# Queries with keys and state sums in all four corners of TensorE, and three of the steps around them in other slots

## The reference

```
for t in range(S):
    kt, vt, bt = (k_n[:, :, t], v[:, :, t], beta[:, :, t, None])
    y[:, :, t] = np.einsum('bhd,bhde->bhe', q[:, :, t], state)
    v_old = np.einsum('bhde,bhd->bhe', state, kt)
    state = state + bt[:, :, :, None] * np.einsum('bhd,bhe->bhde', kt, vt - v_old)
...
h = x @ w_in
g = np.maximum(0.01 * h, h)
x = (g @ w_out)
...
e_idx = np.argmax(logits, axis=1)
out[mask] = gate_w[mask, None] * (np.maximum(x[mask] @ w1[e], 0.0) @ w2[e])
```

## Time and profile before

| | |
|---|---|
| median of three runs | 981.32 us |
| the three runs | 974.87, 981.32, 982.77 us |
| profiled execution | 978.93 us |
| its span, first to last instruction | 977.2 us |
| mean granted clock of PE | 0.957 |
| PE busy | 870.9 us |
| DVE busy | 553.5 us |
| ACT busy | 350.6 us |
| DMA, mean | 80 GB/s |

### The profile page before, as it was taken

The page is one execution under the profiler, slowest core; times in us unless marked ns, Lnnn a source line. Parts: engine busy times, 40 slices in busy tenths (PEclk is TensorE's granted clock), DMA queues, the critical chain, the costliest instruction groups (busy, mean ns, idle before and its releaser), DMA issues.

```text
span 977.2 us, 26906 instructions
## 1 busy us (share of the span) xinstructions
PE 870.9 (89%) x10528; PEld 766.0 (78%) x10529; DVE 553.5 (57%) x1578; ACT 350.6 (36%) x609; POOL 87.6 (9%) x100
## 2 busy tenths in 40 slices
PE   3775889989999998999989999999969999999962
PEld 3664678878888887888878888888759898889862
DVE  4974994588638862798359842344642333333350
ACT  3364335542545253444444342323411212121230
POOL 1000000000020002000100001010121212121210
PEclk9965899999999999999999999999999999999996
DMA  9904272345143533344153313255051111111122
GB/s 127 337 4 75 62 150 68 68 107 101 34 92 74 104 62 52 99 86 81 41 102 84 74 28 84 58 94 175 32 171 33 48 32 48 32 48 32 40 74 73
DMA packets 148308, 77.92 MB, mean 80 GB/s; under 512 B 112496, under 2 KB 144240, under 8 KB 147824
## 3 DMA queue, kind: packets, MB, share of 16 engines
q1 hardware_dynamic: 143264, 66.59, 30.4%
q0 software_dynamic: 4096, 9.48, 3.2%
q10 hardware_dynamic: 848, 0.39, 0.2%
HBM read 59.30 MB, written 13.21 MB: 74 GB/s over the span
## 4 chain that ended last, share of the span: by engine, by line
PE 67%; DVE 15%; ACT 7%; DMA 4%; issue 3%; SPq 1%; ACTq 1%; DVEq 0%; POOL 0%; POOLq 0%
PE bank L518 17%; PE bank L503 14%; PE bank L605 11%; PE bank L580 10%; DVE inv_t L1299 2%; DVE inv_tmp L1293 2%; PE bank L590 2%; PE bank L381 2%; PE bank L410 2%; ACT diag L987 2%; DVE g_raw L1368 1%; PE bank L484 1%; DVE tr L1305 1%; PE bank L471 1%; DVE inv_a L1255 1%
## 5 line engine op out<-in xcount | busy, mean ns | idle before, releaser
L518 PE MATMUL bank<-wo_hi,g_hi 128*128 128x392 f32 x384 | 139.1, 362 | 7.3 <-DVE g_lo L1373 4.0
L518 PE MATMUL bank<-wo_hi,g_lo 128*128 128x392 f32 x384 | 132.2, 344 | 0.0
L518 PE MATMUL bank<-wo_lo,g_hi 128*128 128x392 f32 x384 | 132.1, 344 | 0.0
L1368 DVE SCALAR_TENSOR_TENSOR g_raw<-g_raw 128x512 f32<-128x512 f32 x96 | 66.3, 691 | 105.0 <-ACT g_raw L1043 105.0
L503 PE MATMUL bank<-x_hi,wi_hi 128*128 128x512 f32 x288 | 118.3, 411 | 6.2 <-ACT g_raw L1043 3.4
L1043 ACT ACTIVATE g_raw<-bank 128x512 f32<-128x512 f32 x96 | 57.3, 597 | 170.5 <-PE bank L503 170.1
L503 PE MATMUL bank<-x_hi,wi_lo 128*128 128x512 f32 x288 | 114.0, 396 | 0.0
L503 PE MATMUL bank<-x_lo,wi_hi 128*128 128x512 f32 x288 | 113.9, 395 | 0.0
L1050 ACT ACTIVATE g_hi<-g_raw 128x512 fp32r<-128x512 f32 x96 | 60.7, 632 | 116.9 <-DVE g_raw L1368 116.9
L1373 DVE TENSOR_TENSOR g_lo<-g_raw,g_hi 128x512 fp32r<-128x512 f32 x96 | 66.3, 691 | 41.9 <-ACT g_hi L1050 41.7
L518 PEld LDWEIGHTS bank<-wo_hi,g_hi 128*128 128x128 f32 x384 | 72.7, 189 | 13.8 <-issue 6.0
(11 more groups left out here) (215 smaller groups left out, 1493.3 us busy)
## 6 DMA issues: line engine op xcount, KB each, us to landing
wo_lo<-wo_lo_d SPq DMA_DIRECT2D x80, 196.0 KB, 2.4
w_raw<-in_moe_w SPq DMA_DIRECT2D x6, 1536.0 KB, 8.4
x_rows<-stage SPq DMA_DIRECT2D x6, 770.0 KB, 6.2
kq_in_rows<-in_k SPq DMA_DIRECT2D x6, 768.0 KB, 7.0
k_raw<-in_k SPq DMA_DIRECT2D x24, 192.0 KB, 4.0
vals<-in_v SPq DMA_DIRECT2D x48, 96.0 KB, 2.9
kq_in_rows<-in_q SPq DMA_DIRECT2D x6, 768.0 KB, 8.8
x_raw<-y_t SPq DMA_DIRECT2D x33, 96.0 KB, 2.4
```

What stands on the lines that cost most here:

```text
L518: mm = pe.matmul(acc[i][:, 0:DX], g[f % 2][:, P * i:P * i + P], w, start=(f == 0 and k == 0), stop=(f == FT - 1 and k == 2))
L1368: dve.scalar_tensor_tensor(out=g_raw[f % 2][:], in0=g_raw[f % 2][:], scalar=0.01, in1=g_raw[f % 2][:], op0=ALU.mult, op1=ALU.max).then_inc ...
```

## The change

- `gram_q(t, c)` does the 16 pairs of a chunk in one go, into two banks, in four corners; it stands in slot 15 (chunk 0) and at the head of slot 0, ahead of `up(n, 1)` (chunk 1), instead of slots 15, 0, 1 and 2.
- `state_sum(t, c)` does its 16 pairs in one go, in four corners; that of chunk 1 stands ahead of `down` in slot 12, where there was one half ahead of it and one behind.
- Odd pairs' results now lie in the other half of the partitions. So for odd pairs `mask_q` and `add_s` take two DVE instructions of 64 partitions each, which read one half of the bank and write the other half of the tile.
- `add_s` of chunk 1 stands ahead of `norm` on DVE, `mask_q` of chunk 1 in slot 0.
- The queries' third and fourth transposes stand behind `down` in slot 13 instead of in slot 14, and their copies behind the first two on ACT.

```diff
--- before.py
+++ after.py
@@ -400,16 +400,17 @@
                                       beta_rows[:, c, :, :].rearrange("p a b -> p (a b)"), ident[:PAIRS, :PAIRS])
                 mm.then_inc(s.beta_tp, 1)
 
-            def gram_q(t, m):
-                for i in range(2):
-                    pe.wait_ge(*is_drained(("QT", t, m % 2 * 2 + i)))
-                b, done = fill(("QK", t, m))
+            def gram_q(t, c):
+                for m in range(4):
+                    pe.wait_ge(*is_drained(("QT", t, m)))
+                to = [fill(("QK", t, c, odd)) for odd in range(2)]
                 for j in range(8):
-                    pair = m % 2 * 8 + j
-                    for hh in range(2):
-                        mm = pe.matmul(b[half_p(hh), CH * j:CH * j + CH], k_t[head_p(hh), pair, chunk(m // 2)],
-                                       q_t[head_p(hh), pair, chunk(m // 2)], start=True, stop=True)
-                mm.then_inc(done, 1)
+                    for odd in range(2):
+                        for hh in range(2):
+                            mm = pe.matmul(to[odd][0][half_p(hh ^ odd), CH * j:CH * j + CH], k_t[head_p(hh), 2 * j + odd, chunk(c)],
+                                           q_t[head_p(hh), 2 * j + odd, chunk(c)], start=True, stop=True)
+                        if j == 7:
+                            mm.then_inc(to[odd][1], 1)
 
             def merge_x(t, m):
                 pe.wait_ge(s.tr_ready, t + 1)
@@ -459,22 +460,24 @@
                         if j == 7:
                             mm.then_inc(to[odd][1], 1)
 
-            def state_sum(t, c, m):
-                if c == 0 and m == 0:
+            def state_sum(t, c):
+                if c == 0:
                     pe.wait_ge(s.k_in, 64 * t + 64)
                 for odd in range(2):
                     pe.wait_ge(*is_drained(("U", t, c, odd)))
-                b, done = fill(("S", t, c, m))
+                to = [fill(("S", t, c, odd)) for odd in range(2)]
                 for j in range(8):
-                    g = 16 * c + 8 * m + j
-                    for hh in range(2):
-                        mm = pe.matmul(b[head_p(hh), HD * j:HD * j + HD], k_raw[half_p(hh), g, :], u_sb[half_p(hh), g, :],
-                                       start=True, stop=True)
-                mm.then_inc(done, 1)
+                    for odd in range(2):
+                        g = PAIRS * c + 2 * j + odd
+                        for hh in range(2):
+                            mm = pe.matmul(to[odd][0][head_p(hh ^ odd), HD * j:HD * j + HD], k_raw[half_p(hh), g, :], u_sb[half_p(hh), g, :],
+                                           start=True, stop=True)
+                        if j == 7:
+                            mm.then_inc(to[odd][1], 1)
 
             def outputs(t, c):
                 for m in range(2):
-                    pe.wait_ge(*is_drained(("QK", t, 2 * c + m)))
+                    pe.wait_ge(*is_drained(("QK", t, c, m)))
                     pe.wait_ge(*is_drained(("U", t, c, m)))
                 to = [fill(("Y", t, c, odd)) for odd in range(2)]
                 for j in range(8):
@@ -614,14 +617,14 @@
 
             def slot(n, f):
                 cur, nxt, ff = is_set(n + 1), is_set(n + 2), n >= 0
+                if cur and f == 0:
+                    gram_q(n + 1, 1)
                 if ff and f < FT - 1:
                     up(n, f + 1)
                 if n == -1 and f == 13:
                     pe.wait_ge(s.beta_cp, 1)
                     up(0, 0)
                 if cur:
-                    if f < 3:
-                        gram_q(n + 1, f + 1)
                     if f == 5:
                         merge_x(n + 1, 0)
                         merge_x(n + 1, 1)
@@ -641,16 +644,13 @@
                     if f == 11 and n >= 0:
                         outputs(n + 1, 1)
                     if f == 12:
-                        state_sum(n + 1, 1, 0)
+                        state_sum(n + 1, 1)
                 if n >= 1 and f == (3 if n == TT - 1 else 8):
                     ranks(n - 1)
                 if nxt:
                     if f == 13:
                         queries_t(n + 2, 0)
                         queries_t(n + 2, 1)
-                    if f == 14:
-                        queries_t(n + 2, 2)
-                        queries_t(n + 2, 3)
                     if f == 15:
                         gram_q(n + 2, 0)
                 if n == -1 and f == 4:
@@ -668,10 +668,7 @@
                     if f == 5 and n >= 0:
                         old_values(n + 1, 0)
                     if f == 7:
-                        state_sum(n + 1, 0, 0)
-                        state_sum(n + 1, 0, 1)
-                    if f == 12:
-                        state_sum(n + 1, 1, 1)
+                        state_sum(n + 1, 0)
                 if nxt:
                     if f == 8:
                         keys_t(n + 2, 0)
@@ -685,6 +682,9 @@
                         gram_k(n + 2, 0)
                     if f == 11:
                         gram_k(n + 2, 1)
+                    if f == 13:
+                        queries_t(n + 2, 2)
+                        queries_t(n + 2, 3)
 
             pe.wait_ge(s.ident_rdy, 1)
             pe.wait_ge(s.pads_zero, 1)
@@ -1305,10 +1304,16 @@
                 dve.transpose(tr[:].rearrange("p g c -> p c g"), inv_t[:].rearrange("p i c -> p c i")).then_inc(s.tr_ready, 1)
                 dve.transpose(diag[:].rearrange("p g i -> p i g"), inv_t[:]).then_inc(s.tt_ready, 1)
 
-            def mask_q(t, m):
-                dve.wait_ge(*is_filled(("QK", t, m)))
-                dve.tensor_tensor(qk_t[:, eight(m), :], by_8(att_bank(("QK", t, m))[:]),
-                                  mask[:].unsqueeze(1).broadcast_to([P, 8, CH]), ALU.mult).then_inc(drain(("QK", t, m)), 1)
+
+            def halves(odd):
+                return [(half_p(hh), half_p(1 - hh)) for hh in range(2)] if odd else [(slice(0, P), slice(0, P))]
+
+            def mask_q(t, c, odd):
+                dve.wait_ge(*is_filled(("QK", t, c, odd)))
+                for to, at in halves(odd):
+                    mm = dve.tensor_tensor(qk_t[to, every_other(c, odd), :], by_8(att_bank(("QK", t, c, odd))[at, :]),
+                                           mask[at, :].unsqueeze(1).broadcast_to([to.stop - to.start, 8, CH]), ALU.mult)
+                mm.then_inc(drain(("QK", t, c, odd)), 1)
 
             def scale_v(t):
                 dve.wait_ge(s.v_in, 128 * t + 128)
@@ -1333,10 +1338,12 @@
                 x = vals[:, every_other(c, odd), :]
                 dve.tensor_tensor(x, x, by_48(att_bank(("W", t, c, odd))), ALU.subtract).then_inc(drain(("W", t, c, odd)), 1)
 
-            def add_s(t, c, m):
-                dve.wait_ge(*is_filled(("S", t, c, m)))
-                old, new = (state[i][:, eight(m), :].rearrange("p a b -> p (a b)") for i in (c, 1 - c))
-                dve.tensor_tensor(new, old, att_bank(("S", t, c, m))[:, 0:8 * HD], ALU.add).then_inc(drain(("S", t, c, m)), 1)
+            def add_s(t, c, odd):
+                dve.wait_ge(*is_filled(("S", t, c, odd)))
+                old, new = state[c], state[1 - c]
+                for to, at in halves(odd):
+                    mm = dve.tensor_tensor(new[to, odd::2, :], old[to, odd::2, :], by_48(att_bank(("S", t, c, odd))[at, :]), ALU.add)
+                mm.then_inc(drain(("S", t, c, odd)), 1)
 
             def split_wi(p):
                 dve.wait_ge(s.wih, p + 1)
@@ -1547,14 +1554,16 @@
                 for i in inv[:len(inv) // 2]:
                     inverse(inv_set, i)
                 if cur:
-                    if f < 3:
-                        mask_q(n + 1, f + 1)
+                    if f == 0:
+                        mask_q(n + 1, 1, 0)
+                        mask_q(n + 1, 1, 1)
                     if f == 5:
                         copy_x(n + 1, 0)
                     if f == 8:
                         sub_w(n + 1, 1, 0)
                 if nxt and f == 15:
-                    mask_q(n + 2, 0)
+                    mask_q(n + 2, 0, 0)
+                    mask_q(n + 2, 0, 1)
                 if ff and f < FT - 1:
                     rest_g(n, f + 1)
                 if 0 <= n < TT - 1 and f == 14:
@@ -1571,6 +1580,9 @@
                         add_s(n + 1, 0, 1)
                     if f == 8:
                         sub_w(n + 1, 1, 1)
+                if cur and f == 12:
+                    add_s(n + 1, 1, 0)
+                    add_s(n + 1, 1, 1)
                 if nxt:
                     if f == 10:
                         copy_gram(n + 2, 0, 1)
@@ -1580,9 +1592,6 @@
                         if n == -1:
                             split_x(0)
                         norm(n + 2)
-                if cur and f == 12:
-                    add_s(n + 1, 1, 0)
-                    add_s(n + 1, 1, 1)
                 for i in inv[len(inv) // 2:]:
                     inverse(inv_set, i)
                 if cur and f == 4:
```

## The result

| | before | after |
|---|---|---|
| median | 981.32 us | 985.82 us |
| lowest to highest of 15 runs | 973.99 to 985.42 | 980.79 to 992.01 |
| ratio, with its 95% interval | | 1.0066 [1.0037, 1.0095] |
| span of the profiled execution | 977.2 us | 979.1 us |
| mean granted clock of PE | 0.957 | 0.940 |

The kernel is 0.7% slower, some 6.5 us by the ratio. The two profiled executions differ by 1.9 us of span alone, but the expert layer, which the change doesn't touch, took 282.1 us in the one after and 285.1 in the one before; the layer begins at 692.2 us before and at 697.0 after. So up to there the profiles show 4.9 us. The profiled execution of the kernel after took 980.79 us, the lowest of its 15, so its profile can show less than the usual loss.

What follows compares the result with a forecast made beforehand. PE and DVE were taken as both nearly full, DVE with thin reserve. Terms 2.2 - 2.45 - 0.85 + 1.8 + 0.2 + 2.5 = +3.4 us gave 982.3 or 984.7, taken as 983 us; range 972 to 990.

Steps and rivals of the forecast that it cites:

- The mechanism: Sets 2 to 5, slot 12 to inverse end: PE's 5 us a set turns into waits, DVE loses its idle time.
- The walk through set 3: Slot-by-slot timing from slot 12 to `tr`: the stretch gets 0.54 us longer, though PE works 5 us less.
- The price of half instructions: DVE masks and additions: each half costs full price without overlap; masks +1.8 us a set, additions +0.74 us a chunk.
- no hold: Rival: DVE half instructions overlap like others; -1.4 us in all, 977.5 us; chance 0.17.
- double price: Rival: DVE half instructions that cross halves cost double, 5 us a set more, above 1000 us; chance 0.04.
- set 1's, +2.5 us: Inverse of set 1, where DVE works without pause: masks add 1.8 us and additions 0.74, together +2.5.
- What followed set 1: From set 1's `tr` to set 2's additions: a change of -0.49 us.
- the gain in slot 7: Chunk 0 state sums in four corners take 1.08 us instead of 1.57: -0.49 in each of five sets, -2.45.
- The clock rival: Rival: PE waits in slots 13 to 0 lower the granted clock; once a set 989 us, twice 996; chance 0.13.
- PE's saving: Rival that it comes through: some 4.6 us for each of four sets, -17 in all, 962 us; chance 0.08.
- The four stretches of inverse in sets 2 to 5: Slot 12 to the end of the inverse: 0.54 us longer each, +2.2 us for four sets.

Runs made afterwards that it cites:

- one full mask: Changed kernel with the odd pairs' mask as one 128-partition instruction without swapping halves, leaving that output part wrong: 991.1 us, ratio 1.0009.
- none of the halves: Changed kernel with odd pairs' masks and state additions each one 128-partition instruction without swapping halves, output partly wrong: 1036.99 us, ratio 1.0459.
- set 1 alone in the old order: Changed kernel with `gram_q` of chunk 1 behind `up` in slot 0 of the first tile only, ahead of it elsewhere: 1001.62 us, ratio 1.0085.
- the state's part alone: Kernel before with only state sums in four corners and half-instruction additions; chunk 1's additions ahead of `norm`: ratio 1.0013; behind it: 0.9996.
- The doubled products: Changed kernel with every `gram_q` matmul done twice into the same place, output unchanged: 1004.92 us, ratio 1.0140.
- second profile: Profile of the changed kernel run again with no edit, on another chip: 1002.08 us, ratio 1.0106.

## Why the prediction was nearly right

The forecast was 983 us and no change that can be told; 985.82 was measured, inside the range, and the loss is small but shown. Step by step:

- **The mechanism held.** In the pattern set DVE has no idle time ahead of `leaky` in slots 0 to 3, where it had some before; PE waits 2.08 us ahead of a transpose in slot 13 (forecast 2) and 1.03 us for a mask (forecast about 0.9), and up to 1.7 us for `g_lo` (forecast 1.7). The walk through set 3 gave 6.62, 4.42, 4.05 and 3.90 us for the slots; 6.57, 4.33, 3.96 and 4.08 came. From addition to `tr` it gave 46.00 us; 46.03 came. With one full mask or none of the halves, the same slots are 1.7 us shorter.
- **The price of half instructions held.** 2.1 us for three masks was forecast and 2.10 measured; 1.68 for three additions, 1.71 measured. Crossing halves costs nothing above that: 64x512 takes 688 ns in the mean and 128x512 684. Two additions started 0.47 us apart before; of three, the second and third start 0.59 and 0.56 behind the one ahead. The rivals of no hold and of double price fall by these rows. The chain of set 1 shows the hold: the first of three masks adds 0.60 us behind the instruction ahead of it, which it overlaps, and the two halves add 0.69 and 0.68. This agrees with the Trainium skill, "VectorE: DVE Perf Modes", section "Two Vector instructions with no wait between them": an instruction that starts in another quadrant is held until those ahead have finished.
- **The term that failed is set 1's, +2.5 us.** It priced DVE's extra instructions only (1.8 for masks, 0.74 for additions). I walked through the banks for set 3 and found 0.9 us for the mask; set 1 got no walk. There DVE is further behind PE, and PE stood 5.5 us ahead of `gram_q` with `up(0, 1)` behind it. From `norm` to `tr` +4.6 us came instead of +1.8. The kernel with set 1 alone in the old order confirms the place: 43.0 us from `norm` to `tr` where the changed one beside it took 46.2.
- **What followed set 1 was missed as well.** From its `tr` to set 2's additions the time is 58.3 us against 56.4, where -0.49 was forecast. It holds the stretch 148 to 154.8 us at a granted clock of 0.52, which costs 6.8 x 0.48 = 3.3 us of PE at full speed.
- **Outside, the gain in slot 7 was undersized.** I took 1.08 us for the state sums in four corners. The chain shows

```profile
167.30 0.87 PE bank L473 x64
```

  so the gain is 0.70 a burst and not 0.49 (the earlier trace rows has 1.57). That is 1.8 times as fast; the Trainium skill, "TensorEngine Tiling (Array Packing)", section Overview, has up to 2x. The missed 0.21 us in each of five sets is too little to be seen: the state's part alone measured 1.0013 and 0.9996.
- **The clock rival came too, at its place, but not in the first profile.** There 306 to 346 us, with pauses of 2.08 and 1.03 us, stay at 1.00, and the lower level shows around set 1: 0.50 from 106.9 to 120.4 us, where it had fallen before the 5.5 us wait began, and 0.52 behind the inverse of that set. In the profiles from later chips it falls in slot 13 behind the 2.1 us wait, where I had argued it, in 12 of 15 sets. I had priced a fall at 1.7 us; it costs 1.0 to 1.6. So the chance of 0.13 was too low for those chips.
- **PE's saving did not come through**, as forecast, and for the reason forecast: in these slots the time follows DVE. The doubled products and the full mask show it in numbers, where the prediction had argued it from reserves. Where DVE is relieved, the saving does come, 1.9 us a set from `x_lo` to `tr`.

The sum, at the start of the expert layer: forecast +3.4, in the profiles +4.9. Up to set 1's `norm` 2.2 came of 2.7. The inverse of set 1 gave 2.8 us more than forecast and the piece behind it 2.4 more. The four stretches of inverse in sets 2 to 5 gave +1.6 in place of +2.2. The rest gave -5.4 in place of -2.8, but 4.0 us of that lie between sets 3 and 4, where the execution before had a pause of PE and a lower clock behind it that the one after had not. So two errors partly took each other away, which is luck. With the missed terms alone the sum would have been 3.4 + 2.8 + 2.4 = 8.6; the ratio's +6.5 us lies between that and the +4.9 of the profiles.

Open stays how much of the loss is the lower clock. The changed kernel has 10.2 us of it between 120 and 640 us in the first profile and 20.4 in the second; the kernel before has 6.8, the kernel with one full mask 34 and measures as fast as the one before. So a count of such stretches in one execution is no measure of a kernel, and the clock alone doesn't make the changed kernel slower than the one before. But each fall in slot 13 costs its 1.0 to 1.6 us, the kernel before showed none there, and how often it falls in a usual execution no run shows. Open stays also why the same change costs 0.66% in the first pair and 1.06% on another chip: that second profile has one such fall (1.6 us) and longer pauses, which doesn't add up to the difference for certain.

## What to carry to other kernels

Before packing matmuls tighter, look at who drains them: if the packing puts results in other partitions, each odd instruction of the draining engine splits in two at full price each, and where that engine has only 0.3 to 0.8 us of reserve in a stretch of 5, that can cost as much as the packing saves or more. Price the exchange per stretch and not per engine total; the cheap test is to double the work on the one engine and to halve it on the other, and see which of the two the time follows. A merged step needs all its inputs at once, and what stands behind it waits with it, 5.5 us in set 1 here; that another place for it saves time was not shown beyond the noise (2 us of 990). Walk its waits in the first stretch, where the pipeline isn't full, and not only in the steady one. And compare kernels by stretches between two fixed instructions: from `x_lo` to `tr` the changed kernel repeats within 0.1 us on two chips, while the whole of it takes 986 us on one and 1002 on the other.

## What the runs showed that I hadn't expected

**Stalls inside `outputs`.** Runs of small matmuls have pauses with no releaser in the profile, and in its second profile, from another chip, the same kernel has more of them. The changed kernel, in the first profile and the second:

```profile
PE bank L491 <- issue: 2.1, 3, 1.3
```

```profile
PE bank L491 <- issue: 5.1, 9, 1.6
```

The last set shows what may come with them. The part behind its inverse took 61.8 us in the first and 68.3 in the second, for the same instructions:

```profile
559.00:620.80 61.80, 59.91 (x1116) 52.52 (x1115) 29.54 (x52) 25.55 (x39) 3.87 (x4) 1.00 0.25 63
```

```profile
568.70:637.00 68.30, 63.97 (x1117) 55.54 (x1116) 29.52 (x53) 25.43 (x39) 3.88 (x4) 0.95 0.22 57
```

PE was idle 2.4 us more and busy 4.1 us more, at a granted clock of 0.95. In the kernel before, the granted clock fell behind such a pause too, of 2.49 us: from 388 to 391.4 us it is 0.53.

```profile
388.00:391.40 3.40, 3.40 (x56) 2.94 (x58) 0.00 (x0) 0.04 (x1) 0.00 (x0) 0.53 0.30 29
```
